# Attention value product: three query groups per head pair joined to two, with the output transposes moved later

## The chip, the cores and the metric

One Trainium2 chip; the kernel runs on one core. The metric is device microseconds (us) of one execution. The engines of a core run side by side and meet only at semaphores: PE (TensorE: matmul, and transpose as a matmul against an identity), PEld (its weight loads), DVE (VectorE), ACT (ScalarE), POOL (GpSimd) and SP (SyncE, which here issues the DMA transfers).

## The reference

Three layers in a row: an attention with pooled queries, a soft mixture of experts, and a gated feed-forward layer. Only the first is touched.

```
B, H, S, D = q.shape                      # 4, 8, 1152, 64
q_pool = q.reshape(B, H, S // 2, 2, D).mean(axis=3)        # 576 queries a head
scores = scale * np.matmul(q_pool, k.transpose(0, 1, 3, 2))  # 576 x 1152
scores = scores - np.max(scores, axis=-1, keepdims=True)
attn = np.exp(scores)
attn = attn / (np.sum(attn, axis=-1, keepdims=True) + 1e-09)
return np.matmul(attn, v).astype(np.float32)               # 576 x 64
```

What follows (2304 tokens of 512 features through the experts and the feed-forward layer) reads the whole attention output.

## The kernel before

The 32 heads are worked off as 16 pairs of heads. A pair has 2 x 576 queries. Eight score tiles hold 128 queries of one head each; the ninth holds the last 64 queries of both heads. So `NTILE` is 9, and one pass over a pair (`pair`) has nine periods, t = 0 to 8, of three chunks j = 0 to 2. In this document (t, j) is a chunk, and a prime, as in (0', 2), means the next pair's pass.

PE's order is written out by hand in `pair` (the loop that calls `job`, `score_chunk` and `weighted`). In each chunk it does

- `job`: three 128 x 128 transposes of a softmax tile that is two periods old, into one of two PSUM banks of `tbank` that all jobs take in turn; a job waits until the job two before it has been copied out;
- `score_chunk`: the scores of the tile of period t against 384 keys, two matmuls (four in period 8, whose tile has queries of both heads). Chunk 0 waits for the exponential of tile t - 2, chunk 2 for that of tile t - 1;
- in chunk 1 only, an extra job of the table `EXTRA`: K0, K1, Q0 and KQ transpose keys and queries of the next pair; O0 (four transposes) and O1 (one) transpose the finished output of the pair before;
- in chunk 1 only, after that, a burst of value matmuls (`weighted`) of the table `PV`.

DVE copies the transposed probabilities of chunk 1 to the tile `pt` (or `pt_tail`), divides what O0 and O1 transposed by the row sums into `x_nat` (`normalise`, lines 852 and 856), and takes the row maxima of the scores: one pass over chunks 0 and 1 (`maxima`, line 806), one over chunk 2 (`maxima_end`, line 813). ACT copies the probabilities of chunks 0 and 2 (line 746), takes the exponential of the tile of the period before (`softmax_exp`, line 718), and copies finished value sums from the PSUM bank `obank` to `o_t` (`copy_group`, line 733). In period 3 DVE has four small operations more (`inverses`).

The value product of a pair, transposed, is (64 values x 576 queries) for each head; the two heads lie in partitions 0 to 63 and 64 to 127 of `obank`. It is done in three groups of queries: group 0 (256 queries), group 1 (256) and group 2 (the last 64). Each sums over nine key tiles, so it takes 18 matmuls in the program, and as the data is plain 32-bit float each of them is two matmul instructions in the trace: 36 a group. A group is spread over several periods. `PV` counts periods through: 6, 7, 8 are periods of the pair itself, 9 to 14 are periods 0 to 5 of the next pair's pass. There is one `obank`: the first burst of a group waits until ACT has copied the group before out, and until the last transposed tile that it needs has been copied to `pt`.

One cycle of value work therefore runs from period 6 of a pair to period 5 of the next pair's pass. After the last pair there is one more pass (`ends=(NPAIR,)`) without scores, here called the drain. It does the last two transposed tiles, the rest of the last pair's value work, O0 and O1. Then a barrier for all engines ends the phase, and the experts begin.

The keys and queries of the next pair reach the score matmuls by DMA copies (`stack`) that SP issues after KQ has been worked up by ACT and POOL; the scores of (0', 0) wait for the first head's copies, those of (1', 0) for the second's.

Of the kernel before, what the change touches and what calls it, by code (L numbers as in the profile page):

```python
# [6 lines left out]
P = 128  # L7
FP32 = mybir.dt.float32
# [78 lines left out]

EXTRA = {(1, 1): "K0", (2, 1): "K1", (3, 1): "Q0", (4, 1): "KQ", (5, 1): "O0", (7, 1): "O1"}  # L90
PREPS = ("K0", "K1", "Q0", "KQ")
PREP_BY_ACT = ("K0", "K1", "Q0", "KQ")
JOBS = []
# [33 lines left out]
def in_range(pair, k):  # L127
# [2 lines left out]

PV = {6: (0, (0, 1, 2)), 7: (0, (3, 4)), 8: (0, (5, 6)), 9: (0, (7, 8)),
      10: (1, (0, 1, 2)), 11: (1, (3, 4, 5)), 12: (1, (6, 7, 8)),
      13: (2, (0, 1, 2, 3, 4)), 14: (2, (5, 6, 7, 8))}

s_scores = Stream(3 * NTILE, in_range)
s_tiles = Stream(NTILE, in_range)
s_jobs = Stream(len(JOBS), job_exists)
s_by_act = Stream(len(JOBS), lambda p, k: job_exists(p, k) and job_by_act(k))  # L140
s_by_dve = Stream(len(JOBS), lambda p, k: job_exists(p, k) and not job_by_act(k))
s_groups = Stream(3, in_range)


def previous_user(at, k, back=2):
# [22 lines left out]
def attention(nc, mem, q, k, v):  # L168
# [24 lines left out]
    v_in = sb("v_in", [P, 2, 2, NK * D], FP32)  # L193
    probs = sb("probs", [P, 2, S], FP32)
    pt_at = mem.at
    pt = sb("pt", [P, 2, 2, NK, 2 * P], FP32)
    pt_tail = sb("pt_tail", [P, NK, P], FP32)
    o_t = sb("o_t", [P, 2, SQ], FP32)
    one = sb("one", [P, 1], FP32)
    row_max = sb("row_max", [P, 2, 2], FP32)  # L200
# [9 lines left out]
    mem.at = pt_at + 4 * 2 * NK * 2 * P  # L210
    q_parts = sb("q_parts", [P, 2, NI, 3, D], F32R)
    q_total = sb("q_total", [P, 2, NI, D], FP32)
    assert mem.at <= pt_at + 4 * 4 * NK * 2 * P
    mem.at = after_pt
    scores = ps("scores", [P, 5, 512])
    tbank = ps("tbank", [P, 2, 512])
# [166 lines left out]
    @block.sync  # L383
    def _(sp):
        def load_keys(at, ahead):
            par = (at.pair + ahead) % 2
            two = bass.ds(at.index(ahead) * 2, 2)
            if at.pair + ahead == 1:
                sp.wait_ge(q_parts_v, 2)
                sp.wait_ge(q_parts_p, 3)  # L390
            else:
                for h in range(2):
                    sp.dma_start(k_in[:, par, :, h, :], k_v[:, bass.ds(at.index(ahead) * 2 + h, 1)].rearrange(
                        "p n j d -> p (n j) d")).then_inc(k_loaded[par], 16)
                sp.wait_ge(q_pooled, pooled(at, ahead - 1))
            sp.dma_start(q_in[:, :, 0:NF, :].rearrange("p h i m -> p h (i m)"),
                         q_full[:, two, :]).then_inc(q_loaded[par], 16)
            sp.dma_start(q_in[0:TAIL, :, NF, :], q_tail[:, two, :]).then_inc(q_loaded[par], 16)

        def load_values(at, ahead):  # L400
            par = (at.pair + ahead) % 2
            two = bass.ds(at.index(ahead) * 2, 2)
            sp.dma_start(v_in[:, par], v_v[:, two, :]).then_inc(v_loaded[par], 16)

        for h in range(2):
            sp.dma_start(k_stage[:, h].rearrange("p j d -> p (j d)"), k_v[:, h].rearrange("p j d -> p (j d)")
                         ).then_inc(k_staged[h], 16)
            sp.dma_start(q_in[:, h, 0:NF, :].rearrange("p i m -> p (i m)"),
                         q_full[:, h, :]).then_inc(q_loaded[0] if h else q_first_in, 16)
        sp.dma_start(q_in[0:TAIL, :, NF, :], q_tail[:, 0:2, :]).then_inc(q_loaded[0], 16)  # L410
        for h in range(2):
            sp.dma_start(k_in[:, 1, :, h, :], k_v[:, 2 + h]).then_inc(k_loaded[1], 16)
        load_keys(At(0), 1)
        load_values(At(0), 0)
        load_values(At(0), 1)

        def body(at):
            last = extra_at("KQ")
            if at.pair + 2 < NPAIR:

                if at.pair >= 1:
                    sp.wait_ge(job_ready, s_jobs.count(at, 1, last))
                load_keys(at, 2)
            if at.pair + 1 < NPAIR:


                sp.wait_ge(lo_ready, split_count(at, 1, "KQ"))
                stack(sp, at, 1)
                if at.pair >= 1:

                    sp.wait_ge(group_ready, s_groups.count(at, 1, 2))
                    load_values(at, 1)
            if at.step is None and at.pair == 1:
                for n in range(EARLY):
                    mem.load_weight(sp, n)

        each_pair(sp, body)

        for par in range(2):
            for h in range(2):  # L440
                sp.wait_ge(stacked[par][h], 16 * HEAD_DMAS[h] * (NPAIR // 2 - (par == 0)))
        mem.load_weight(sp, 2)

        sp.wait_ge(scores_ready, 3 * NTILE * (NPAIR - 1))
        mem.load_weight(sp, 3)
        mem.load_weight(sp, 4)
        sp.wait_ge(scores_ready, 3 * NTILE * NPAIR)
        mem.load_weight(sp, 5)
# [47 lines left out]
    def _(pe):  # L496
# [5 lines left out]
        def job(at, k):  # L502
            kind, period, j = JOBS[k]
            if not job_exists(at.pair, k):
                return
            user = previous_user(at, k)

            if user is not None:
                back, e = user
                if job_by_act(e):  # L510
                    pe.wait_ge(out_by_act, s_by_act.count(at, back, e))
                else:
                    pe.wait_ge(out_by_dve, s_by_dve.count(at, back, e))
            elif bank_of(at, k):
                pe.wait_ge(first_by_act, 5)
            else:
                pe.wait_ge(first_by_dve, 1)
            if kind == "main" and j == 0:
                back, t = tile_of(at.pair, period)
                pe.wait_ge(exp_done, s_tiles.count(at, back, t))  # L520
            if kind == "K0":
                pe.wait_ge(k_loaded[(at.pair + 1) % 2], loads(at, 1) * 32)
            if kind == "Q0":
                pe.wait_ge(q_pooled, pooled(at, 1))
            if kind == "O0":
                pe.wait_ge(group_out, s_groups.count(at, 1, 1))
            if kind == "O1":
                pe.wait_ge(group_out, s_groups.count(at, 1, 2))
            transposes(at, k, bank_of(at, k))

        def score_chunk(at, t, c):
# [35 lines left out]
        def weighted(at, back, group, tiles):  # L567
# [3 lines left out]
            par = (at.pair - back) % 2  # L571
            if tiles[0] == 0:

                last_tile = (3, 7, 8)[group]
                period = last_tile + 2
                b2, per = (back, period) if period < NTILE else (back - 1, period - NTILE)
                for j in (1, 2):
# [3 lines left out]
                    else:  # L581
                        pe.wait_ge(out_by_dve, s_by_dve.count(at, b2, e))

                g = 3 * (at.pair - back) + group
                if g >= 1:
                    b3, gg = (back, group - 1) if group else (back + 1, 2)
                    pe.wait_ge(group_out, s_groups.count(at, b3, gg))
                else:
                    pe.wait_ge(first_by_dve, 7)
                if group == 0:  # L590
                    pe.wait_ge(v_loaded[par], (uses(at, -back)) * 16)
            for kt in tiles:
                for h in range(2):
                    rows = slice(D * h, D * h + D)
                    if group < 2:
                        rhs, cols = pt[:, group, h, kt, :], slice(0, 2 * P)
                    else:
                        rhs, cols = pt_tail[:, kt, TAIL * h:TAIL * h + TAIL], slice(0, TAIL)
                    last = nc.tensor.matmul(obank[rows, cols], v_in[:, par, h, D * kt:D * kt + D],  # L599
                                            rhs, start=(kt == 0), stop=(kt == NK - 1))  # L600
            if tiles[-1] == NK - 1:
                last.then_inc(group_ready, 1)

# [72 lines left out]
    def pt_out(at, k):  # L676

        _, period, j = JOBS[k]
        back, t = tile_of(at.pair, period)
        parity = (NTILE * (at.pair - back) + t) % 2  # L680
        first = key_tile(parity, 3 * j)
        if t == 2 * NF:
            return pt_tail[:, first:first + 3, :]
        i, h = divmod(t, 2)
        return pt[:, i // 2, h, first:first + 3, P * (i % 2):P * (i % 2) + P]

    def pt_free(engine, at, k):

        _, period, j = JOBS[k]
        back, t = tile_of(at.pair, period)  # L690
        group = 2 if t == 2 * NF else t // 4
        if at.pair - back >= 1:
            engine.wait_ge(group_ready, s_groups.count(at, back + 1, group))

# [1 line left out]
    def _(act):  # L696
# [26 lines left out]
        def copy_group(at, back, group):  # L723
# [5 lines left out]

            if group == 0 and at.pair - back >= 2:  # L730
                act.wait_ge(job_ready, s_jobs.count(at, back + 1, extra_at("O1")))
            first, n = ((0, 2 * P), (2 * P, 2 * P), (NF * P, TAIL))[group]
            nc.scalar.copy(o_t[:, par, first:first + n], obank[:, 0:n]).then_inc(group_out, 1)

        def pair(at):
            for t in range(NTILE):

                for period, back, group in ((1, 1, 0), (4, 1, 1), (6, 1, 2)):
                    if t == period:
                        copy_group(at, back, group)  # L740
                for j in range(3):
                    e = JOBS.index(("main", t, j))
                    if job_exists(at.pair, e) and job_by_act(e):
                        act.wait_ge(job_ready, job_count(at, e))
                        pt_free(act, at, e)
                        nc.scalar.copy(pt_out(at, e), tbank[:, bank_of(at, e), 0:3 * P].rearrange(  # L746
                            "p (r q) -> p r q", r=3)).then_inc(out_by_act, 1)
                    if j == 0:

                        softmax_exp(at, *((0, t - 1) if t else (1, NTILE - 1)))  # L750
# [11 lines left out]
    def _(dve):  # L762
# [98 lines left out]
        def pair(at):  # L861
            for t in range(NTILE):
                for j in range(3):
                    e = JOBS.index(("main", t, j))
                    if job_exists(at.pair, e) and not job_by_act(e):
                        dve.wait_ge(job_ready, job_count(at, e))
                        pt_free(dve, at, e)
                        nc.vector.tensor_copy(pt_out(at, e), tbank[:, bank_of(at, e), 0:3 * P].rearrange(  # L868
                            "p (r q) -> p r q", r=3)).then_inc(out_by_dve, 1)
                    if (t, j) in EXTRA:  # L870
                        kind = EXTRA[t, j]
                        e = JOBS.index((kind, t, j))
# [1060 lines left out]
```

## Time and profile before

| | us |
|---|---|
| median of 3 runs | 820.52 |
| lowest, highest | 820.22, 822.13 |
| the profiled execution | 822.02 |
| its span, first to last instruction | 820.0 |
| PE busy in the span | 795.1 |
| DVE busy | 497.2 |
| ACT busy | 462.4 |
| POOL busy | 182.9 |

In the timeline below, a row merges neighbouring instructions of one kind: start, duration from the first start to the last end, engine, line, operation, tiles, shape, count. In square brackets stand the idle time of the engine before the row and what ended it. The ends of matmuls overlap what follows, so the cost of a piece of PE work is read from its start to the start of the next row, not from its duration.

### The profile page before, as it was taken

Reading aid. Unit: us, or ns where it says so; the run is one execution under the profiler, and the core shown is the slowest. Engines: PE = TensorE matmul, PEld = TensorE weight load, DVE = VectorE, ACT = ScalarE, POOL = GpSimd, SP = SyncE. Lnnn points to the kernel's source line nnn. Section 1 sums busy time; section 2 is a strip of 40 time slices with the busy share of each in tenths; the row PEclk is TensorE's granted clock in tenths of the full one; section 3 lists DMA queues with packets and bytes.
Section 4 is the critical chain, followed back from the end, with each engine's and each line's share of the span. In section 5 each row is a group of like instructions: output and inputs, shape, how many; then the busy total and the mean of one; then the engine's idle time right before and its main releaser. Section 6 shows DMA issues by size and latency. Waiting matters only on the chain. (4 is left out here: it accounts for less than half of the span.)

```text
span 820.0 us, 17518 instructions
## 1 busy us (share of the span) xinstructions
PE 795.1 (97%) x5858; PEld 606.6 (74%) x5858; DVE 497.2 (61%) x968; ACT 462.4 (56%) x889; POOL 182.9 (22%) x246
## 2 busy tenths in 40 slices
PE   8999999999999999999999999998799999999997
PEld 7777777777777777777777777765334788888886
DVE  6666657657566666665765766743323566666665
ACT  5676666767666667666676766642123453343333
POOL 4541331513315225133151330000002330000000
PEclk9999999999999999999999999999799899999999
DMA  5738856374382553734637417639799001010110
GB/s 150 182 80 260 225 122 158 78 169 105 96 197 63 143 124 85 194 86 116 158 78 166 107 39 198 255 112 394 301 393 392 5 1 52 0 52 1 51 52 26
DMA packets 83033, 112.05 MB, mean 137 GB/s; under 512 B 45360, under 2 KB 47408, under 8 KB 82480
## 3 DMA queue, kind: packets, MB, share of 16 engines
q1 hardware_dynamic: 82832, 111.24, 47.6%
q8 instruction: 26, 0.43, 0.2%
q10 hardware_dynamic: 160, 0.26, 0.1%
q14 instruction: 15, 0.12, 0.0%
HBM read 71.37 MB, written 4.72 MB: 93 GB/s over the span
## 5 line engine op out<-in xcount | busy, mean ns | idle before, releaser
L562 PE MATMUL scores<-k_stack,q_stack 128*128 128x384 f32 x960 | 275.1, 376 | 2.3 <-DVE q_stack L777 1.2
L499 PE MATMUL tbank<-ident,probs 128*128 128x128 f32 x1296 | 219.6, 278 | 2.8 <-DVE pt L868 2.4
L746 ACT COPY pt<-tbank 128x384 f32<-128x384 f32 x256 | 122.7, 479 | 143.9 <-PE tbank L499 142.7
L499 PEld LDWEIGHTS tbank<-ident,probs 128*128 128x128 f32 x1296 | 156.4, 140 | 58.7 <-issue 40.4
L718 ACT ACTIVATE probs<-scores,neg_max 128x1152 f32<-128x1152 f32 x144 | 175.9, 1221 | 6.5 <-PE tbank L499 2.1
L813 DVE TENSOR_REDUCE row_max<-scores 128x1 f32<-128x384 f32 x144 | 80.0, 556 | 130.1 <-PE scores L562 128.2
L562 PEld LDWEIGHTS scores<-k_stack,q_stack 128*128 128x128 f32 x960 | 147.9, 191 | 3.7 <-ACT k_stack L372 1.6
L599 PE MATMUL obank<-pt,v_in 128*64 128x256 f32 x1152 | 148.8, 389 | 0.0
L806 DVE TENSOR_REDUCE row_max<-scores 128x1 f32<-128x768 f32 x144 | 136.7, 949 | 4.4 <-PE scores L562 1.7
L599 PEld LDWEIGHTS obank<-pt,v_in 128*64 128x64 f32 x1152 | 72.8, 136 | 49.3 <-issue 23.5
L337 POOL TENSOR_TENSOR k_hi<-k_lo,one 128x512 fp32r<-128x512 f32 (+1 forms) x45 | 37.2, 826 | 291.4 <-ACT k_lo L670 270.8
L1698 ACT CAST h_hi<-hid 128x512 fp32r<-128x512 f32 (+1 forms) x60 | 34.7, 578 | 101.2 <-DVE hid L1835 101.2
L868 DVE COPY pt<-tbank 128x384 f32<-128x384 f32 x128 | 71.3, 557 | 32.0 <-PE tbank L499 28.7
L1601 PE MATMUL banks<-wo_hi,h_hi 128*128 128x512 f32 x216 | 85.8, 397 | 0.6 <-DVE h_lo L1841 0.4
L1601 PE MATMUL banks<-wo_lo,h_hi 128*128 128x512 f32 x216 | 84.7, 392 | 0.0
L1601 PE MATMUL banks<-wo_hi,h_lo 128*128 128x512 f32 x216 | 84.5, 391 | 0.0
L1841 DVE TENSOR_TENSOR h_lo<-hid,h_hi 128x512 fp32r<-128x512 f32 (+1 forms) x60 | 38.3, 639 | 37.9 <-ACT h_hi L1698 37.9
L1786 DVE TENSOR_TENSOR scaled<-banks,inv_rms 128x512 f32<-128x512 f32 (+1 forms) x60 | 38.2, 636 | 26.7 <-PE banks L1513 26.0
L1601 PEld LDWEIGHTS banks<-wo_hi,h_hi 128*128 128x128 f32 x216 | 40.9, 190 | 11.3 <-DVE h_lo L1841 3.2
L1601 PEld LDWEIGHTS banks<-wo_hi,h_lo 128*128 128x128 f32 x216 | 40.8, 189 | 8.7
L1601 PEld LDWEIGHTS banks<-wo_lo,h_hi 128*128 128x128 f32 x216 | 40.9, 189 | 8.0
L342 POOL TENSOR_TENSOR k_lo<-k_lo,k_hi 128x512 fp32r<-128x512 f32 (+1 forms) x45 | 45.1, 1003 | 3.5
(220 smaller groups left out, 773.6 us busy)
## 6 DMA issues: line engine op xcount, KB each, us to landing
weights<-in_moe_w SPq DMA_DIRECT2D x7, 2048.0 KB, 9.4
v_in<-in_v SPq DMA_DIRECT2D x16, 576.0 KB, 3.9
k_in<-in_k SPq DMA_DIRECT2D x30, 288.0 KB, 4.8
k_stack<-k_hi SPq DMA_DIRECT2D x30, 288.0 KB, 3.7
k_stack<-k_lo SPq DMA_DIRECT2D x30, 288.0 KB, 3.6
q_in<-in_q SPq DMA_DIRECT2D x15, 512.0 KB, 4.7
slots_of_four<-in_moe_w SPq DMA_DIRECT2D x12, 512.0 KB, 11.2
q_stack<-q_hi SPq DMA_DIRECT2D x30, 144.0 KB, 3.3
```

Of the source, the lines that this page charges most:

```text
L342: last = ops.tensor_tensor(low[:, cols], low[:, cols].bitcast(FP32), high[:, cols].bitcast(FP32), ALU.subtract)
L499: last = nc.tensor.transpose(tbank[:, bank, cols], src, ident[0:rows, 0:rows])
L562: last = nc.tensor.matmul(scores[:, bank, 0:CH], q_stack[at.par][:, h, order, cols], k_stack[at.par][:, h, keys], start=(x == 0), stop=(x ...
L599: last = nc.tensor.matmul(obank[rows, cols], v_in[:, par, h, D * kt:D * kt + D], rhs, start=(kt == 0), stop=(kt == NK - 1))
L718: nc.scalar.activation(probs[:, odd, :].rearrange("p (c k) -> p c k", c=3), scores[:, first:first + 3, 0:CH], ACT.Exp, bias=neg_max[:, odd ...
L746: nc.scalar.copy(pt_out(at, e), tbank[:, bank_of(at, e), 0:3 * P].rearrange("p (r q) -> p r q", r=3)).then_inc(out_by_act, 1)
L806: nc.vector.tensor_reduce(row_max[:, odd, 0:1], scores[:, first:first + 2, 0:CH], axis=AX.XY, op=ALU.max).then_inc(partial_max, 1)
L813: nc.vector.tensor_reduce(row_max[:, odd, 1:2], scores[:, 2, 0:CH], axis=AX.X, op=ALU.max).then_inc(partial_max, 1)
L868: nc.vector.tensor_copy(pt_out(at, e), tbank[:, bank_of(at, e), 0:3 * P].rearrange("p (r q) -> p r q", r=3)).then_inc(out_by_dve, 1)
L1601: last = nc.tensor.matmul(y_ps[:, t, :], a[:, f % 3, cols], w[:, f, :], start=(f == 0 and x == 0), stop=(f == NFT - 1 and x == 2))
L1786: nc.vector.tensor_tensor(scaled[:, f % 2, 0:width], gv_ps[:, f % 2, 0, 0:width], inv_rms[:, columns(n)], ALU.mult).then_inc(scaled_done, 1)
L1841: nc.vector.tensor_tensor(h_lo[:, f % 3, 0:width], hid2[:, f % 2, 0:width], h_hi[:, f % 3, 0:width].bitcast(FP32), ALU.subtract).then_inc( ...
```

## The change

Groups 1 and 2 become one: group 1 now has 320 queries (the former 256 and the last 64), and its matmuls are 320 columns wide. The tile `pt_tail` goes; the probabilities of the last 64 queries are copied to the last 64 columns of group 1's tile, so that the copy out of `tbank` writes two 64-column pieces a key tile instead of 128 columns in a row. ACT copies two groups a pair out of `obank` (256 and 320 columns) instead of three, in periods 2 and 6 instead of 1, 4 and 6. O0 moves from period 5 to 7, O1 from 7 to 8. The bursts are laid out anew:

| period | before: group, matmul instructions | after |
|---|---|---|
| 6 | 0, 12 | 0, 12 |
| 7 | 0, 8 | 0, 8 |
| 8 | 0, 8 | none |
| 0' | 0, 8 | 0, 8 |
| 1' | 1, 12 | 0, 8 |
| 2' | 1, 12 | 1, 12 of 320 columns |
| 3' | 1, 12 | 1, 8 of 320 columns |
| 4' | 2, 20 of 64 columns | 1, 8 of 320 columns |
| 5' | 2, 16 of 64 columns | 1, 8 of 320 columns |

```diff
-EXTRA = {(1, 1): "K0", (2, 1): "K1", (3, 1): "Q0", (4, 1): "KQ", (5, 1): "O0", (7, 1): "O1"}
+EXTRA = {(1, 1): "K0", (2, 1): "K1", (3, 1): "Q0", (4, 1): "KQ", (7, 1): "O0", (8, 1): "O1"}
...
-PV = {6: (0, (0, 1, 2)), 7: (0, (3, 4)), 8: (0, (5, 6)), 9: (0, (7, 8)),
-      10: (1, (0, 1, 2)), 11: (1, (3, 4, 5)), 12: (1, (6, 7, 8)),
-      13: (2, (0, 1, 2, 3, 4)), 14: (2, (5, 6, 7, 8))}
+PV = {6: (0, (0, 1, 2)), 7: (0, (3, 4)), 9: (0, (5, 6)), 10: (0, (7, 8)),
+      11: (1, (0, 1, 2)), 12: (1, (3, 4)), 13: (1, (5, 6)), 14: (1, (7, 8))}
+GROUP_FIRST, GROUP_WIDTH = (0, 2 * P), (2 * P, 2 * P + TAIL)
...
-    pt = sb("pt", [P, 2, 2, NK, 2 * P], FP32)
-    pt_tail = sb("pt_tail", [P, NK, P], FP32)
+    pt = [sb(f"pt{g}", [P, 2, NK, GROUP_WIDTH[g]], FP32) for g in range(2)]
...
-                last_tile = (3, 7, 8)[group]
+                last_tile = (3, NTILE - 1)[group]
...
-                    if group < 2:
-                        rhs, cols = pt[:, group, h, kt, :], slice(0, 2 * P)
-                    else:
-                        rhs, cols = pt_tail[:, kt, TAIL * h:TAIL * h + TAIL], slice(0, TAIL)
-                    last = nc.tensor.matmul(obank[rows, cols], v_in[:, par, h, D * kt:D * kt + D],
-                                            rhs, start=(kt == 0), stop=(kt == NK - 1))
+                    last = nc.tensor.matmul(obank[rows, 0:GROUP_WIDTH[group]], v_in[:, par, h, D * kt:D * kt + D],
+                                            pt[group][:, h, kt, :], start=(kt == 0), stop=(kt == NK - 1))
...
         if t == 2 * NF:
-            return pt_tail[:, first:first + 3, :]
+            return pt[1][:, :, first:first + 3, 2 * P:2 * P + TAIL].rearrange("p h r q -> p r h q")
...
-                for period, back, group in ((1, 1, 0), (4, 1, 1), (6, 1, 2)):
+                for period, back, group in ((2, 1, 0), (6, 1, 1)):
```

The waits on group 2 become waits on group 1; the rest of the diff counts groups as two instead of three.

## Rows read from the trace of the kernel before

**Rows 1.** The page's busy time of each engine, share of the span, instructions.

```profile
PE 795.1 (97%) x5858; PEld 606.6 (74%) x5858; DVE 497.2 (61%) x968; ACT 462.4 (56%) x889; POOL 182.9 (22%) x246
```

**Rows 2.** All of PE's waits, 60 to 525 us: total, times, longest.

```profile
PE tbank L499 <- DVE pt L868: 2.4, 12, 0.2
```

**Rows 3.** Timeline of PE, period 0' to chunk (1', 0) of the first cycle.

```profile
39.60 0.49 PE L499 MATMUL tbank<-ident,probs 128*128 128x128 f32 x3
40.28 0.49 PE L499 MATMUL tbank<-ident,probs 128*128 128x128 f32 x3
...
42.81 0.49 PE L499 MATMUL tbank<-ident,probs 128*128 128x128 f32 x3
43.75 0.62 PE L562 MATMUL scores<-k_stack,q_stack 128*128 128x384 f32 x2 [0.45 <-DMA q_stack<-q_lo]
```

**Rows 4.** Timeline of PE, periods 4 to 8 of a later pass.

```profile
223.71 0.80 PE L599 MATMUL obank<-pt_tail,v_in 128*64 128x64 f32 x20
224.71 0.55 PE L499 MATMUL tbank<-ident,probs 128*128 128x128 f32 x3 [0.20 <-DVE pt L868]
...
226.82 0.60 PE L499 MATMUL tbank<-ident,o_t 128*128 128x128 f32 x4
...
230.15 1.51 PE L599 MATMUL obank<-pt,v_in 128*64 128x256 f32 x12
231.60 0.55 PE L499 MATMUL tbank<-ident,probs 128*128 128x128 f32 x3
...
233.70 0.27 PE L499 MATMUL tbank<-ident,o_t 128*128 128x128 f32 x1
233.90 1.08 PE L599 MATMUL obank<-pt,v_in 128*64 128x256 f32 x8
234.92 0.55 PE L499 MATMUL tbank<-ident,probs 128*128 128x128 f32 x3
...
235.66 0.49 PE L499 MATMUL tbank<-ident,probs 128*128 128x128 f32 x3
...
236.69 0.49 PE L499 MATMUL tbank<-ident,probs 128*128 128x128 f32 x3
```

**Rows 5.** Timeline of DVE and ACT in the same stretch.

```profile
227.59 0.69 DVE L852 TENSOR_TENSOR x_nat<-tbank,row_inv 128x512 f32 x1 [0.37 <-PE tbank L499]
...
234.14 0.29 DVE L856 TENSOR_TENSOR x_nat<-tbank,tail_inv 64x128 f32 x1
234.46 0.96 DVE L806 TENSOR_REDUCE row_max<-scores 128x1 f32<-128x768 f32 x1
...
235.86 0.56 DVE L813 TENSOR_REDUCE row_max<-scores 128x1 f32<-128x384 f32 x1 [0.44 <-PE scores L562]
236.19 0.48 ACT L746 COPY pt<-tbank 128x384 f32<-128x384 f32 x1 [0.20 <-PE tbank L499]
...
236.70 1.22 ACT L718 ACTIVATE probs<-scores,neg_max 128x1152 f32<-128x1152 f32 x1
...
237.21 0.56 DVE L868 COPY pt<-tbank 128x384 f32<-128x384 f32 x1 [0.55 <-PE tbank L499]
...
237.82 0.19 ACT L718 ACTIVATION_READ_ACCUMULATOR probs<-scores,neg_max 128x1 f32 x1
```

**Rows 6.** Timeline of all engines in the drain.

```profile
540.93 1.52 PE L599 MATMUL obank<-pt,v_in 128*64 128x256 f32 x12
...
545.71 0.37 ACT L733 COPY o_t<-obank 128x256 f32<-128x256 f32 x1 [2.27 <-PE obank L599]
...
546.23 0.80 PE L599 MATMUL obank<-pt_tail,v_in 128*64 128x64 f32 x20 [0.56 <-ACT o_t L733]
546.96 0.66 PE L499 MATMUL tbank<-ident,o_t 128*128 128x128 f32 x4
547.72 0.69 DVE L852 TENSOR_TENSOR x_nat<-tbank,row_inv 128x512 f32<-128x512 f32 x1 [5.44 <-PE tbank L499]
548.97 0.29 DVE L856 TENSOR_TENSOR x_nat<-tbank,tail_inv 64x128 f32<-64x128 f32 x1 [0.56 <-PE tbank L499]
```

More of the change, by code:

```diff
@@ L141 @@
 s_by_dve = Stream(len(JOBS), lambda p, k: job_exists(p, k) and not job_by_act(k))
-s_groups = Stream(3, in_range)
+s_groups = Stream(2, in_range)
 def previous_user(at, k, back=2):
@@ L212, in attention @@
     q_total = sb("q_total", [P, 2, NI, D], FP32)
-    assert mem.at <= pt_at + 4 * 4 * NK * 2 * P
+    assert mem.at <= pt_at + 4 * 2 * NK * (2 * P + 2 * P + TAIL)
     mem.at = after_pt
@@ L429, in body @@
                 if at.pair >= 1:
-                    sp.wait_ge(group_ready, s_groups.count(at, 1, 2))
+                    sp.wait_ge(group_ready, s_groups.count(at, 1, 1))
                     load_values(at, 1)
@@ L527, in job @@
             if kind == "O1":
-                pe.wait_ge(group_out, s_groups.count(at, 1, 2))
+                pe.wait_ge(group_out, s_groups.count(at, 1, 1))
             transposes(at, k, bank_of(at, k))
@@ L582, in weighted @@
                         pe.wait_ge(out_by_dve, s_by_dve.count(at, b2, e))
-                g = 3 * (at.pair - back) + group
+                g = 2 * (at.pair - back) + group
                 if g >= 1:
-                    b3, gg = (back, group - 1) if group else (back + 1, 2)
+                    b3, gg = (back, 0) if group else (back + 1, 1)
                     pe.wait_ge(group_out, s_groups.count(at, b3, gg))
@@ L682, in pt_out, with pt_from @@
         if t == 2 * NF:
-            return pt_tail[:, first:first + 3, :]
+            return pt[1][:, :, first:first + 3, 2 * P:2 * P + TAIL].rearrange("p h r q -> p r h q")
         i, h = divmod(t, 2)
-        return pt[:, i // 2, h, first:first + 3, P * (i % 2):P * (i % 2) + P]
+        return pt[i // 2][:, h, first:first + 3, P * (i % 2):P * (i % 2) + P]
+    def pt_from(at, k):
+        cells = tbank[:, bank_of(at, k), 0:3 * P]
+        if tile_of(at.pair, JOBS[k][1])[1] == 2 * NF:
+            return cells.rearrange("p (r h q) -> p r h q", r=3, h=2)
+        return cells.rearrange("p (r q) -> p r q", r=3)
     def pt_free(engine, at, k):
@@ L690, in pt_free @@
         back, t = tile_of(at.pair, period)
-        group = 2 if t == 2 * NF else t // 4
+        group = min(t // 4, 1)
         if at.pair - back >= 1:
@@ L731, in copy_group @@
                 act.wait_ge(job_ready, s_jobs.count(at, back + 1, extra_at("O1")))
-            first, n = ((0, 2 * P), (2 * P, 2 * P), (NF * P, TAIL))[group]
+            first, n = GROUP_FIRST[group], GROUP_WIDTH[group]
             nc.scalar.copy(o_t[:, par, first:first + n], obank[:, 0:n]).then_inc(group_out, 1)
@@ L745, in pair @@
                         pt_free(act, at, e)
-                        nc.scalar.copy(pt_out(at, e), tbank[:, bank_of(at, e), 0:3 * P].rearrange(
-                            "p (r q) -> p r q", r=3)).then_inc(out_by_act, 1)
+                        nc.scalar.copy(pt_out(at, e), pt_from(at, e)).then_inc(out_by_act, 1)
                     if j == 0:
@@ L867, in pair @@
                         pt_free(dve, at, e)
-                        nc.vector.tensor_copy(pt_out(at, e), tbank[:, bank_of(at, e), 0:3 * P].rearrange(
-                            "p (r q) -> p r q", r=3)).then_inc(out_by_dve, 1)
+                        nc.vector.tensor_copy(pt_out(at, e), pt_from(at, e)).then_inc(out_by_dve, 1)
                     if (t, j) in EXTRA:
```

## Prediction

> **What bounds the kernel now.** I read the page's busy times first. PE is busy 97% of the span, DVE 61%, ACT 56% [rows 1]. A busy PE need not be an unbroken one, so I then asked for PE's waits over the 465 us in which the passes are all alike: 12 waits of 0.2 us, 2.4 us together, all for one DVE copy [rows 2]. The reader is to see what is not there: no wait for ACT, POOL or DMA. DVE and ACT wait for PE instead (the idle times in [rows 5] end with PE). So until the drain the time is the sum of PE's own work in its written order, and an edit is worth what it takes from that order, plus that wait, unless it creates a wait. Last I read PE's timeline, where work is measured from start to start, and the drain, where PE does wait.
>
> **The change part by part.**
>
> *Cost of a burst.* A chunk of three transposes and two score matmuls takes 0.68 us without a burst (39.60 to 40.28 [rows 3]). Chunks (0, 1) and (0, 2) with a burst of 8 between them take 40.28 to 42.81 = 2.53 us [rows 3]; less 2 x 0.68, that burst costs 1.17 us. One of 12 lasts 230.15 to 231.60 = 1.45, one of 8 233.90 to 234.92 = 1.02 [rows 4]: 0.1075 us for each further 256-column matmul. So a burst costs 1.17 - 8 x 0.1075 = 0.31 us beside its matmuls, 0.16 of it inside the burst (1.02 - 8 x 0.1075). Eight bursts instead of nine: -0.31 us a cycle.
>
> *Cost of the columns.* The tail's burst of 20 lasts 546.23 to 546.96 = 0.73 us [rows 6], so a 64-column matmul costs (0.73 - 0.16) / 20 = 0.0285. The trace has no 320-column matmul. On the line through the 64- and 256-column values it costs 0.1075 + 64 x (0.1075 - 0.0285) / 192 = 0.134. I take that: it is the same operation on the same operands. The lower end is 0.1075 (the 64 columns for nothing). For the upper end I take the worst column rate on this engine: period 8's chunk, with two more 384-column score matmuls, takes 235.66 to 236.69 = 1.03 [rows 4] against 0.68, so 0.175 each, which gives 0.146 for 320. With 36 instructions of each kind: 36 x (0.1075 + 0.0285 - 0.134) = 0.07 us less a cycle, between 1.0 less and 0.36 more.
>
> *Cycles.* 15 full cycles (the 16th ends in the drain): 15 x (0.31 + 0.07) = 5.7 us less.
>
> *The wait that goes.* In period 4 the tail's burst takes 223.71 to 224.71 = 1.00 us instead of 0.73, because chunk (4, 2) waits for DVE's copy of (4, 1), late behind DVE's extra operations of period 3 [rows 4]. After, the burst there is 8 matmuls of 320 columns, 8 x 0.134 + 0.16 = 1.23 us, longer than what DVE needs, so the wait is covered. 12 waits [rows 2] x 0.27 = 3.2 us less. What is late next is nothing on PE: the next exponential has the longer bursts of periods 4 and 5 as cover.
>
> *O0 and O1 moved.* Four transposes and one take the same PE time wherever a burst or a chunk follows; their row durations, 0.60 and 0.27 [rows 4], differ by 0.11 us a transpose. But period 8 loses its burst, the cover for DVE's work, and DVE's longer division (0.69 us, 227.59) takes the place of the short one (0.29, 234.14) just before [rows 5]. Followed with the trace's times: the burst of period 7 starts 0.33 later, (7, 2) at 235.25, (8, 0) at 235.99, (8, 1) at 237.02. With no burst (8, 2) follows after 1.03 + 0.11, at 238.16, and can score after its three transposes, at 238.40; its scores need the exponential of tile 7. DVE divides O0 from 234.47 to 235.16 (0.77 after the transposes, as at 226.82 and 227.59), takes the maxima to 236.13 and reaches the second pass at 236.19, when the scores of (7, 2) are ready (235.86 + 0.33). The exponential starts 0.84 later (as 236.70 after 235.86), at 237.03, and is through 1.31 later (237.82 + 0.19 - 236.70), at 238.34. ACT's copy of (8, 0) moves by the same 0.33 and is out of its way. That is 0.06 us ahead of need. The copy of (8, 1) that (8, 2) needs ends at 238.10, also 0.06 ahead. O1's division then pushes the maxima of tile 8; the same steps give its exponential at 241.92, and (0', 2) needs it at 241.97. Three margins of 0.05 us are less than the hand-over between engines is known to. I charge 0.07 us a cycle: 15 x 0.07 = 1.0 us more. The lower end is 0; the upper is 0.40, by which O0's division is longer than O1's, were nothing of it hidden: 6.0 us.
>
> *The first cycle.* Here chunk (1', 0) waits 0.45 us for the stacked queries of pair 1 [rows 3]; they come from work done before the first value burst, which the change leaves where it is. PE arrives there 1.17 us earlier (period 8 has no burst) and waits that much longer: +1.2 us. Later passes have no such wait [rows 2].
>
> *Copies.* ACT's copy of 64 columns goes and one of 256 grows to 320; ACT has idle time there. The tail's copies write 64-column pieces. No row shows that shape; at 0.48 (ACT, 236.19) and 0.56 us (DVE, 237.21) [rows 5] for the same 384 elements I cost the change at nothing, from 0.1 less up to a doubling, which DVE's one copy a pass could show at most as 0.56 us in period 1', where an 8-burst of 1.02 lies over it. No DMA is issued earlier or later in SP's order; the value load waits, as before, for the last burst of period 5.
>
> *The drain.* Up to (8, 2) PE is 0.33 - 1.02 = 0.69 us earlier, but tile 8's exponential, which the drain's transposes wait for, only some 0.36 (O1's division lies before it). Then a burst of 8 of group 0 stands where the first of group 1 stood: 540.93 - 0.36 = 540.57 to 541.59. Group 1 now waits until ACT has copied the last transposes (0.48, 0.58 after they start, as for (8, 0)) and group 0 (0.37): to 543.02, and a hand-over of 0.15 (546.08 to 546.23 [rows 6]) makes 543.17. 36 x 0.134 = 4.82 us to 547.99; ACT's copy, 0.26 later and 0.43 long (an estimate from 0.37 for 256 columns), to 548.68; O0 at 548.83, its division 0.76 later (546.96 to 547.72) and 0.69 long, O1's 0.29: 550.6. Before, the end is 548.97 + 0.29 = 549.26 [rows 6]. +1.4 us. The barrier behind it moves by the same, and the phases after it rigidly.
>
> *Sum.* -5.7 - 3.2 + 1.0 + 1.2 + 1.4 = -5.3 us. The profiled execution took 822.02 us (span 820.0), so it becomes 816.7; the median of the runs, 1.5 lower, goes from 820.5 to 815.2.
>
> **A rule against the row.** The tail burst of 20 in 0.73 us [rows 6] holds 20 weight loads as well, so hardly any of a load shows. The Trainium skill ("TensorE: Matmul & The Clock Gate", section "Part 3: Packing small matmuls — row/col tiling") says that a weight load overlaps matmuls in flight only when its row group differs; here all loads use all 128 rows. By that rule and the page's load time, 53 ns for 64 columns (an estimate), dropping 36 loads a cycle would give 1.9 us a cycle, near 30 us in all. The trace disagrees: 0.0285 us a matmul is less than such a load.
>
> **The rivals.**
> (A) *Period 8 becomes bound by DVE and ACT.* The chain maxima, exponential, scores of (8, 2) ends after PE. For it: the margins above. Against: in [rows 5] DVE still waits 0.44 us for PE at 235.86, so O0's extra 0.40 just fits. If 0.25 to 0.40 us shows in each cycle, the time is 817.9 to 820.2.
> (B) *Wide matmuls cost more than their columns.* 320 columns could run like 384, 0.1075 x 1.5 = 0.161. That is 0.027 x 36 = 0.97 us a cycle, over 16 cycles 15.6: 830.8, slower. It turns slower from 0.148 on ((0.1475 - 0.134) x 576 = 7.8 us leads to 823.0), which the score matmuls' rate of 0.146 nearly reaches. Against it: those carry 128-column weights of another type, and 64 and 256 columns of the same operation lie on one line with almost no offset.
> (C) *The wait in period 4 stays*, since DVE, not PE, sets that time. For it: DVE's lateness is unchanged. Against: the new burst is 0.23 us longer than the old one with its wait. Time 815.2 + 3.2 = 818.4.
> (D) *The weight loads that go are worth time.* Even if the last 64 queries came free, the gain would be 36 x 0.0285 = 1.03 us a cycle instead of 0.07, 15.4 us more: 799.8. The short tail matmuls speak against it.
>
> **How the numbers follow.** A measurement here can tell about 0.3%, 2.5 us, from no change: below 818.0 is faster, above 823.0 slower. My forecast 815.2, with its own range 812.5 to 817.5 (a first cycle, drain and stalls that cost 2.7 us less or 2.3 more): 0.72. More gain than that, D with it: 0.05. A: 0.11, of which 0.04 below 818.0. C: 0.06, half of it on either side. B: 0.06, slower. So faster 0.72 + 0.05 + 0.04 + 0.03 = 0.84, same 0.07 + 0.03 = 0.10, slower 0.06. The range reaches up to the lower part of A and to C: 812.3 to 818.5.
>
> **What would show it.** In the changed profile: 320-column matmuls 0.134 us apart (B if 0.146 or more); a cycle 0.65 us shorter; no wait of (4, 2) for DVE (C if it is there); at (8, 2) and (0', 2) waits for ACT of at most 0.1 us each (A if 0.25); a wait for DMA near 1.6 us at the first (1', 0); 1.3 us more from the drain's last group to the barrier. The prediction is wrong if waits of PE that are not listed here come up in every pass.

## The result and the profile after

The changed kernel takes 814.61 us (median of 4 runs, 813.68 to 815.96) against 820.89 for the kernel before on the same chip: a ratio of 0.9917, 95% interval 0.9896 to 0.9937. Forecast were 815.2 us and a gain of 5.3; it is faster by 6.3. The profiled execution took 815.96 us, 6.06 less than the one before.

The page of the changed kernel, busy time of each engine (after [rows 1]):

```profile
PE 788.2 (97%) x5282; PEld 586.0 (72%) x5282; DVE 499.2 (61%) x968; ACT 460.9 (57%) x873; POOL 183.2 (23%) x246
```

576 matmul instructions fewer, 36 for each of 16 cycles, and PE as busy as before. The view of PE's waits from 60 to 525 us ([rows 2]) has no entry left. PE's timeline: two period-7 bursts one pass apart (199.64 and 232.34), the burst before chunk (4, 2), and chunks (8, 1) and (8, 2):

```profile
199.64 1.08 PE L594 MATMUL obank<-pt,v_in 128*64 128x256 f32 x8
...
221.42 1.30 PE L594 MATMUL obank<-pt,v_in 128*64 128x320 f32 x8
222.65 0.55 PE L498 MATMUL tbank<-ident,probs 128*128 128x128 f32 x3
...
232.34 1.08 PE L594 MATMUL obank<-pt,v_in 128*64 128x256 f32 x8
...
235.12 0.49 PE L498 MATMUL tbank<-ident,probs 128*128 128x128 f32 x3
235.37 0.95 PE L561 MATMUL scores<-k_stack,q_stack 128*128 128x384 f32 x4
236.15 0.27 PE L498 MATMUL tbank<-ident,o_t 128*128 128x128 f32 x1
236.26 0.55 PE L498 MATMUL tbank<-ident,probs 128*128 128x128 f32 x3
236.56 0.94 PE L561 MATMUL scores<-k_stack,q_stack 128*128 128x384 f32 x4
```

DVE, ACT and PEld (PE's weight loads) in the same stretches:

```profile
222.03 0.56 DVE L869 COPY pt<-tbank 128x384 f32<-128x384 f32 x1 [0.19 <-DVE tail_inv L838]
...
222.64 0.31 PEld L498 LDWEIGHTS tbank<-ident,probs 128*128 128x128 f32 x3 [0.49 <-DVE pt L869]
...
234.29 0.56 DVE L814 TENSOR_REDUCE row_max<-scores 128x1 f32<-128x384 f32 x1 [0.16 <-PE scores L561]
...
235.65 0.56 DVE L869 COPY pt<-tbank 128x384 f32<-128x384 f32 x1 [0.55 <-PE tbank L498]
...
236.25 0.19 ACT L720 ACTIVATION_READ_ACCUMULATOR probs<-scores,neg_max 128x1 f32 x1
236.26 0.31 PEld L498 LDWEIGHTS tbank<-ident,probs 128*128 128x128 f32 x3
```

A pass is 32.70 us; before it was 33.29. The 8-burst of 320 columns takes 1.23 us, as forecast, and PE loses nothing behind it (before: 1.00 with the wait, [rows 4]). But the cover is only just long enough: DVE's copy of (4, 1) ends at 222.59, 1.17 us after the burst began, and the weight load of (4, 2) that needs it starts 0.05 us later, just when the burst is over.

At (8, 2) the step from transposes to scores is 0.30 us, where (8, 1) has 0.25. These 0.05 us are not the exponential of tile 7. It is through at 236.44, 0.12 us before the scores; in the kernels below whose scores do wait for it, they start 0.05 us after its end. The cause is DVE's copy of (8, 1): with O1's job in between, (8, 2) takes the bank of (8, 1), and the weight load of its first transpose starts at 236.26, 0.05 us after that copy ends (236.21), as at (4, 2).

PE's timeline shortly after the first bursts, the answer to the last two of [rows 3]:

```profile
42.52 0.49 PE L498 MATMUL tbank<-ident,probs 128*128 128x128 f32 x3
44.58 0.62 PE L561 MATMUL scores<-k_stack,q_stack 128*128 128x384 f32 x2 [1.57 <-DMA q_stack<-q_lo]
...
49.90 1.84 PE L594 MATMUL obank<-pt,v_in 128*64 128x320 f32 x12
51.66 0.55 PE L498 MATMUL tbank<-ident,probs 128*128 128x128 f32 x3
```

The wait for the DMA grew from 0.45 to 1.57 us. Over the whole trace a burst of 12 takes 1.77 us on average, a burst of 8 1.23: 0.134 us for each further 320-column matmul. The drain, all engines (after [rows 6]):

```profile
533.49 1.08 PE L594 MATMUL obank<-pt,v_in 128*64 128x256 f32 x8
...
535.47 0.38 ACT L735 COPY o_t<-obank 128x256 f32<-128x256 f32 x1
...
535.99 5.07 PE L594 MATMUL obank<-pt,v_in 128*64 128x320 f32 x36 [0.94 <-ACT o_t L735]
541.09 0.42 ACT L735 COPY o_t<-obank 128x320 f32<-128x320 f32 x1 [5.25 <-PE obank L594]
...
541.66 0.74 PE L498 MATMUL tbank<-ident,o_t 128*128 128x128 f32 x5 [0.61 <-ACT o_t L735]
542.40 0.69 DVE L853 TENSOR_TENSOR x_nat<-tbank,row_inv 128x512 f32<-128x512 f32 x1 [7.55 <-PE tbank L498]
543.12 0.29 DVE L857 TENSOR_TENSOR x_nat<-tbank,tail_inv 64x128 f32<-64x128 f32 x1
...
543.74 2.48 PE L1035 MATMUL banks<-ident,x_nat 128*128 128x128 f32 x21 [1.34 <-PEq L1885]
```

The spans, 820.02 and 813.95 us, cut at instructions of PE that both kernels have:

| stretch | before, us | after, us | difference |
|---|---|---|---|
| start to the first value burst | 29.94 | 30.70 | +0.76 |
| to the scores of pair 2 | 43.75 | 43.41 | -0.34 |
| 13 passes, to the scores of pair 15 | 432.62 | 425.08 | -7.54 |
| to the first matmul of the next phase | 43.28 | 44.55 | +1.27 |
| the next phases | 270.43 | 270.21 | -0.22 |

The first row is no part of the change, whose first edit lies behind it. The same load lands later in this execution, and PE, which waits for it, falls below its upper level of 2.4 GHz. DVE's timeline and the busy times with the granted clock (the column after POOL) of the changed kernel:

```profile
7.87 0.23 DVE L349 TENSOR_TENSOR q_total<-q_in 128x64 f32<-128x64 f32 x1 [2.41 <-DMA q_in<-in_q]
```

```profile
8.00:12.00 4.00, 2.90 (x11) 2.83 (x12) 3.05 (x8) 0.12 (x1) 3.21 (x7) 0.65 0.09 18
```

Before, DVE waited 1.56 us there and the clock was 1.00. In the ten traces of this document the first value burst starts at 29.50 to 30.70 us and the next phases take 267.3 to 271.4, though no edit touches either. So for each kernel below I also give what the change can touch, from the first value burst to the first matmul of the next phase, called the core: 519.65 us before, 513.04 after, 6.61 less.

### The profile page after: what moved, and what is told of

The parts are those of the page before. It is cut to its first block and busy times, and to the rows that moved or that the text cites. A ratio compares the mean times of both kernels' runs of the same rounds, so it can differ in the third digit from the quotient of the medians.

```text
span 814.0 us, 16310 instructions
## 1 busy us (share of the span) xinstructions
PE 788.2 (97%) x5282; PEld 586.0 (72%) x5282; DVE 499.2 (61%) x968; ACT 460.9 (57%) x873; POOL 183.2 (23%) x246
## 5 line engine op out<-in xcount | busy, mean ns | idle before, releaser
L748 ACT COPY pt<-tbank 128x384 f32<-128x384 f32 x288 | 138.2, 480 | 153.7 <-PE tbank L498 153.7
L594 PE MATMUL obank<-pt,v_in 128*64 128x320 f32 (+1 forms) x1152 | 167.3, 417 | 0.9 <-ACT o_t L735 0.9
L869 DVE COPY pt<-tbank 128x384 f32<-128x384 f32 x144 | 80.2, 557 | 39.0 <-PE tbank L498 36.4
```

The source lines that it names most:

```text
L594: last = nc.tensor.matmul(obank[rows, 0:GROUP_WIDTH[group]], v_in[:, par, h, D * kt:D * kt + D], pt[group][:, h, kt, :], start=(kt == 0), ...
L748: nc.scalar.copy(pt_out(at, e), pt_from(at, e)).then_inc(out_by_act, 1)
L869: nc.vector.tensor_copy(pt_out(at, e), pt_from(at, e)).then_inc(out_by_dve, 1)
```

## Experiments

The theory: PE's written order is the time. A burst less gains 0.31 us a cycle less what the uncovered chain of DVE and ACT takes back in period 8, the covered wait 0.27, the columns 0.07. Rivals: the joined group carries the gain; DVE has room anyway; moving the outputs costs or gains by itself. A pass is the mean of nine, from pair 3 to pair 12.

| kernel | pass, us | core, us | median, us | ratio to before (95%) |
|---|---|---|---|---|
| before | 33.29 | 519.65 | 821.77, 821.65 | |
| early row sums | 33.02 | 516.14 | 818.96 | 0.9961 (0.9945 to 0.9977) |
| eight bursts | 32.96 | 516.91 | 819.43 | 0.9974 (0.9959 to 0.9989) |
| both of these | 32.86 | 515.75 | 816.89 | 0.9948 (0.9928 to 0.9967) |
| changed, nine bursts | 33.08 | 518.62 | 818.9 | 0.9977 (0.9963 to 0.9991) |
| changed, again | 32.70 | 512.91 | 813.86 | 0.9902 (0.988 to 0.9924) |
| changed, divided twice | 32.87 | 516.14 | 818.14 | 0.9954 (0.9937 to 0.997) |
| changed, outputs one earlier | 32.78 | 514.13 | 815.56 | 0.9928 (0.9905 to 0.995) |
| changed, ends mended | 32.71 | 511.19 | 812.9 | 0.9896 (0.9873 to 0.9919) |

The first four beside 30 runs of before, the last four on another chip beside 15.

**The wait alone.** The kernel before, with

```diff
-                if t == 3:
+                if t == 2:
                     inverses(at)
```

> The kernel before, with one edit: DVE's four small operations on the row sums run in period 2 instead of 3. Theory (PE's wait of 0.27 us in period 4 comes from these operations alone, and PE is the bound, so the wait is worth what it lasts): no wait of chunk (4, 2) for DVE is left, a pass is 33.0 instead of 33.3 us, and the time is 3.2 to 3.6 us less than before. Rival (DVE's lateness only moves: the copy it delays in period 3, or the next exponential, holds PE up instead): no gain, and another wait of some 0.2 us a pass.

PE's timeline at period 4:

```profile
223.13 0.80 PE L599 MATMUL obank<-pt_tail,v_in 128*64 128x64 f32 x20
223.87 0.55 PE L499 MATMUL tbank<-ident,probs 128*128 128x128 f32 x3
```

The burst takes 0.74 us instead of 1.00; the core is 3.51 us shorter, as expected, and the median 2.8, somewhat less. Half of what the change gained is to be had by moving one call, without joining anything.

**The burst alone.** The kernel before, with

```diff
-PV = {6: (0, (0, 1, 2)), 7: (0, (3, 4)), 8: (0, (5, 6)), 9: (0, (7, 8)),
-      10: (1, (0, 1, 2)), 11: (1, (3, 4, 5)), 12: (1, (6, 7, 8)),
+PV = {6: (0, (0, 1, 2)), 7: (0, (3, 4)), 9: (0, (5, 6)), 10: (0, (7, 8)),
+      11: (1, (0, 1, 2, 3, 4)), 12: (1, (5, 6, 7, 8)),
...
-                for period, back, group in ((1, 1, 0), (4, 1, 1), (6, 1, 2)):
+                for period, back, group in ((2, 1, 0), (4, 1, 1), (6, 1, 2)):
```

> The kernel before, still with three groups and 64-column tail matmuls, but with eight bursts instead of nine: none in period 8; group 0 in 6, 7, 0', 1' (12, 8, 8, 8 instructions), group 1 in 2' and 3' (20 and 16), tail as before; ACT copies group 0 in period 2. Theory (a burst costs 0.31 us beside its matmuls): 15 x 0.31 = 4.7 us less, the first cycle's DMA wait 1.2 us more, the drain some 1.0 more: 2.5 us less than before; the wait of (4, 2) for DVE stays, and a pass is 33.0 us. Rival (a burst costs only its matmuls, and the gain of the change came from the wider matmuls): no gain in a pass, 2.2 us more in all.

The core is 2.74 us shorter, as expected, but by two errors that cancel. The wait did not stay: the burst of 20 takes 0.82 us, so 0.18 of the wait is gone. And the burst gained less than 0.31. The next run tells how much.

**Both.**

> The two edits of the experiments before together: three groups with 64-column tail matmuls, eight bursts, the operations on the row sums in period 2. Theory (the change gained by a burst less and a wait less; the joined group itself is worth 0.07 us a cycle): 5.5 to 6.1 us less than before, within 1.5 us of the changed kernel (814.6); a pass is 32.7 to 32.8 us. Rival (the joined group carries the gain): the changed kernel stays 3 us or more ahead of this.

Missed: 32.86 us a pass, the core 3.90 us shorter and the median 4.9, not 5.5 to 6.1. Against the early row sums alone the burst brings 0.16 us a pass. PE's timeline at (8, 2), with the end of ACT's exponential of tile 7, shows what takes the rest:

```profile
202.90 0.49 PE L499 MATMUL tbank<-ident,probs 128*128 128x128 f32 x3
203.15 0.94 PE L562 MATMUL scores<-k_stack,q_stack 128*128 128x384 f32 x4
...
203.93 0.49 PE L499 MATMUL tbank<-ident,probs 128*128 128x128 f32 x3
204.03 0.19 ACT L718 ACTIVATION_READ_ACCUMULATOR probs<-scores,neg_max 128x1 f32 x1
...
204.28 0.96 PE L562 MATMUL scores<-k_stack,q_stack 128*128 128x384 f32 x4
```

The step from transposes to scores is 0.25 us in (8, 1) and 0.35 in (8, 2): 0.10 us of waiting for the exponential of tile 7, which ends 0.05 us before the scores. Here O1 is transposed in period 7, so PE reaches (8, 2) 0.11 us sooner, and waits. The changed kernel's core is 2.71 us shorter than this one's, between what the two theories said: the joined group with the later outputs is worth more than I thought, though less than the rival needs.

**A ninth burst.** The changed kernel, with

```diff
-PV = {6: (0, (0, 1, 2)), 7: (0, (3, 4)), 9: (0, (5, 6)), 10: (0, (7, 8)),
+PV = {6: (0, (0, 1, 2)), 7: (0, (3, 4)), 8: (0, (5, 6)), 9: (0, (7,)), 10: (0, (8,)),
```

> The changed kernel with a ninth burst: group 0 in periods 6, 7, 8, 0', 1' (12, 8, 8, 4, 4 instructions). Theory (0.31 us a burst): a cycle of 33.0 instead of 32.7 us, 15 x 0.31 = 4.7 us more, the first cycle's DMA wait 0.7 less: 4.0 us more than the changed kernel, 2.3 less than before. Rival (bursts cost only their matmuls): the same time as the changed kernel.

0.38 us more a pass, the core 5.6 more. The rival is out: the matmuls are the same. But not all of it is the burst. Averaged over the passes, the chunk with the burst of period 8 grows by some 0.25 us more than its matmuls; the rest, some 0.14, is the chain once more, behind the short burst of period 0'. PE's timeline:

```profile
208.32 0.65 PE L594 MATMUL obank<-pt,v_in 128*64 128x256 f32 x4
208.90 0.55 PE L498 MATMUL tbank<-ident,probs 128*128 128x128 f32 x3
209.36 0.62 PE L561 MATMUL scores<-k_stack,q_stack 128*128 128x384 f32 x2
```

From transposes to scores 0.46 us, where [rows 4] and the trace after have 0.30 behind a burst (222.65 to 222.95): 0.16 us of waiting, in every second pass; in those between it is 0.08. A burst costs itself, and gives back what the chain would have made PE wait without it.

**The changed kernel again**, beside the next three.

> The changed kernel as it is, beside the next three on the same chip. Both theories: 6 to 7 us less than before, a pass of 32.70 us.

7.8 us less than before by the medians, a little over the range; pass and core as in the first execution.

**More work for DVE in period 7.** The changed kernel, with

```diff
+                nc.vector.tensor_tensor(
+                    spare[:], tbank[:, bank, :].rearrange("p (i h d) -> p i h d", i=NF, h=2),
+                    inv.unsqueeze(3).broadcast_to([P, NF, 2, D]), ALU.mult).then_inc(spare_done, 1)
                 nc.vector.tensor_tensor(
                     x_pair[:, 0:NF], tbank[:, bank, :].rearrange("p (i h d) -> p i h d", i=NF, h=2),
```

> The changed kernel with DVE's division of O0 in period 7 done twice, the first time into a spare tile: 0.69 us more of DVE work before the maxima of tile 7. Theory (without a burst in period 8 the chain maxima, exponential, scores of (8, 2) runs level with PE; DVE's idle 0.16 us before its second pass of tile 7 is all that is left): some 0.5 us of it shows at (8, 2), a pass of 33.2 us, 15 x 0.5 = 7.5 us more than the changed kernel. Rival (DVE, busy 61%, has room for it): the time stays.

0.17 us a pass, not 0.5, and 3.2 us in the core. The rival is out, but my size was wrong. DVE's and PE's timelines:

```profile
199.83 0.69 DVE L855 TENSOR_TENSOR spare<-tbank,row_inv 128x512 f32<-128x512 f32 x1 [0.23 <-PE tbank L500]
200.44 0.68 DVE L858 TENSOR_TENSOR x_nat<-tbank,row_inv 128x512 f32 x1
201.04 0.95 DVE L809 TENSOR_REDUCE row_max<-scores 128x1 f32<-128x768 f32 x1
201.90 0.55 DVE L816 TENSOR_REDUCE row_max<-scores 128x1 f32<-128x384 f32 x1
```

```profile
203.65 0.55 PE L500 MATMUL tbank<-ident,probs 128*128 128x128 f32 x3
204.10 0.97 PE L563 MATMUL scores<-k_stack,q_stack 128*128 128x384 f32 x4
```

DVE's rows overlap: each starts 0.08 to 0.09 us before the one ahead of it ends, so an operation in a queue costs less than its row's duration, here 0.61 for 0.69 and 0.86 for 0.95. DVE's idle 0.16 us before its second pass (234.29 in the changed kernel) is used up, and the first division starts earlier: 0.63 us after O0's transposes instead of 0.77. So the second pass comes only 0.22 us later after the start of (7, 2). Of that, 0.07 was to spare, as the exponential was through 0.12 us before the scores where 0.05 is enough. The rest, 0.15, is what (8, 2) now waits for the exponential: 0.45 us from transposes to scores instead of 0.30.

**The outputs one period earlier.**

```diff
-(7, 1): "O0", (8, 1): "O1"}
+(6, 1): "O0", (7, 1): "O1"}
```

> The changed kernel with O0 in period 6 and O1 in period 7, one period earlier each. Theory (PE's order decides; but O1's transpose in period 8 fills 0.11 us in which PE would wait for the exponential of tile 7): PE waits up to 0.1 us more at (8, 2), a pass of 32.70 to 32.80 us, the drain 0.3 us shorter: from 0.3 less to 1.3 us more than the changed kernel. Rival (moving the outputs by two periods cost something through DVE in periods 7 and 8): 1 us or more faster than the changed kernel, a shorter pass.

0.08 us more a pass, as expected; the core is 1.2 us longer than the changed kernel's, the median 1.7, and the drain did not get shorter. PE's timeline shows 0.35 us from the transposes of (8, 2) to its scores, so PE waits 0.10 for the exponential, as in the experiment with both edits:

```profile
203.62 0.49 PE L498 MATMUL tbank<-ident,probs 128*128 128x128 f32 x3
203.97 0.97 PE L561 MATMUL scores<-k_stack,q_stack 128*128 128x384 f32 x4
```

O0's and O1's transposes cost PE the same in either place (the chunk of period 6 grows by 0.43 us, those of 7 and 8 shrink by 0.32 and 0.11); what is left is (8, 2), 1.16 us instead of 1.09. The run also isolates the join: this kernel and the one with both edits have the same number of bursts and the same wait at (8, 2), and differ by 0.08 us a pass, against 0.07 forecast for the columns. (O0 and DVE's row-sum operations stand in other periods in the two, but no wait of PE in the passes comes from that.)

**The ends mended.** The changed kernel, with

```diff
+PV_FIRST = {6: (0, (0, 1, 2)), 7: (0, (3, 4)), 8: (0, (5, 6)), 9: (0, (7, 8)),
+            11: (1, (0, 1, 2)), 12: (1, (3, 4)), 13: (1, (5, 6)), 14: (1, (7, 8))}
...
+            final = at.pair == NPAIR and group == 1
+            sums = scores[:, 0, :] if final else obank
...
+                    if at.pair == NPAIR and (t, j) == (1, 2):
+                        weighted(at, 1, 1, (0, 1, 2))
+                        weighted(at, 1, 1, (3, 4, 5, 6, 7, 8))
```

> The changed kernel with its two ends mended: the first pair keeps a burst in period 8 (bursts 6, 7, 8, 0', then none in 1'), and in the drain the last group 1 sums in a bank of the scores that is free by then and starts with key tiles 0 to 2 without waiting for ACT's copies of the last chunk and of group 0. Theory: the wait for DMA at the first (1', 0) shrinks from 1.6 to 0.4 us (1.2 us less), PE's wait of 0.9 us in the drain goes (0.9 to 1.0 less): 2.0 us less than the changed kernel, the same 32.70 us pass. Rival (the ends are hidden behind the next phase's DMA, or PE waits elsewhere for the same transfers): the time of the changed kernel.

PE's timeline at the two ends:

```profile
43.50 0.62 PE L563 MATMUL scores<-k_stack,q_stack 128*128 128x384 f32 x2 [0.52 <-DMA q_stack<-q_lo]
...
533.05 5.07 PE L603 MATMUL scores<-pt,v_in 128*64 128x320 f32 x36
```

The DMA wait is 0.52 us and the last group starts without one. The core is 1.72 to 1.85 us shorter than the changed kernel's, as the theory has it; the medians, 812.9 and 813.86, agree in sign, but their intervals overlap. By the trace it is the fastest of these kernels.

## Why the prediction was right

**The bound, and the steps in a pass.** PE's order was the time: each edit's price came out of PE's timeline. Of the pass I forecast -0.31 - 0.07 - 0.27 + 0.07 = -0.58 us (the signs that I listed have 0.65, without the chain's 0.07); measured -0.59. Each term by itself: the wait 0.27 (early row sums), the columns 0.08 (0.134 us a matmul, as forecast), and the burst 0.38 with the ninth put back, of which some 0.14 is the chain's. That leaves 0.25 for the burst, where I had 0.31 less 0.07 for the chain; without the 0.05 us at (8, 2) in the changed kernel it would be 0.30. So these 0.05 us are about what I had charged, but not where I looked first: of the margins of 0.06 that I had worked out, the exponential's held, and the copy's did not, because I had counted from the transposes and not from the weight load ahead of them, which is what waits. That charge came out by luck, since I could not tell it from nothing.

**A cover that held by luck.** I had the new burst of period 4, 1.23 us, as longer than what DVE needs, which was 1.00 before. But DVE needed 1.22 in the changed kernel (221.42 to 222.64), as one of its small operations took 0.56 us instead of 0.33 (the last section shows why). The wait went, with next to nothing to spare.

**What I had not seen.** The outputs' move pays. I took the later O0 and O1 as a risk for DVE. But O1's transpose, in period 8, is work that PE does while it would wait for the exponential; with it back in period 7 the pass is 0.08 longer. Together with the 0.08 of the columns that makes the 0.16 us a pass by which taking the wait and the burst from the kernel before falls short of the change, most of the 2.7 us of the core, where I had expected 1.5 at most.

**Sizes.** The core gained 6.6 us, not 5.3. The drain cost 0.95 us (from the last pair's period-6 burst to the next phase, 21.77 before and 22.72 after), not 1.4: group 0's burst in the drain came 0.64 us earlier (12.47 after that burst instead of 13.11), not 0.36, because DVE's second pass in the last pair did not wait as long behind O1's division as I counted; and ACT's last two copies overlap by 0.10. The wait was worth 3.5 us (early row sums), not 3.2: I had counted the 12 waits in the view and not two shorter ones, 0.12 us each, in pairs 1 and 14. The DMA wait grew by 1.12, against 1.2.

**The rivals.** A (the chain takes over) is not there in the changed kernel: the exponential is 0.07 us ahead of need. It is close, though: PE waits 0.10 us for it with the outputs one period earlier, 0.15 with a second division. B fell with 0.134. C fell, narrowly: no wait of PE is left in period 4. D fell, and with it the reading of the Trainium skill's rule on weight loads ("TensorE: Matmul & The Clock Gate", section "Part 3: Packing small matmuls — row/col tiling") that I weighed: the loads that went were worth at most what the columns' term holds, 0.08 us a cycle.

**Still open.** The 0.76 us at the start and up to some 4 us between executions in the last phases (267.3 to 271.4 us over these traces), which no edit touched, were not looked into beyond the one load above.

## What to carry to other kernels

Where one engine is without waits, price an edit by the steps from start to start on that engine: a burst there cost some 0.25 to 0.31 us beside its matmuls, and fusing two groups was worth far less (0.08) than having a burst less. Such a step can hold a wait shorter than those that the view of waits lists, so compare it with the same step elsewhere, and compare the end of each candidate with the start that it should hold up: 0.05 us apart was a wait here, 0.12 was not. Before a piece of work is taken from such an engine, look at the chain beside it: the piece was cover, and a small independent operation moved into the gap (0.11 us of transpose) can pay for itself. And look for the wait that is one moved call away; it was half of this gain.

## What the runs showed of the hardware

A DVE operation of nine values waited for POOL. The row-sum addition takes 0.16 us in the eight-burst kernel, 0.33 in the kernel before and 0.56 in the changed one; these three timelines show why, before, changed, and eight bursts:

```profile
221.98 1.28 POOL L342 TENSOR_TENSOR q_lo<-q_lo,q_hi 128x512 fp32r<-128x512 f32 x1
...
222.96 0.33 DVE L831 TENSOR_SCALAR row_sum_eps<-row_sum 128x9 f32<-128x9 f32 x1
```

```profile
219.91 1.29 POOL L341 TENSOR_TENSOR q_lo<-q_lo,q_hi 128x512 fp32r<-128x512 f32 x1
...
220.67 0.56 DVE L832 TENSOR_SCALAR row_sum_eps<-row_sum 128x9 f32<-128x9 f32 x1
```

```profile
220.48 1.28 POOL L342 TENSOR_TENSOR q_lo<-q_lo,q_hi 128x512 fp32r<-128x512 f32 x1
...
221.89 0.16 DVE L831 TENSOR_SCALAR row_sum_eps<-row_sum 128x9 f32<-128x9 f32 x1
```

In the first two it ends 0.03 us after POOL's operation ends (223.29 and 223.26; 221.23 and 221.20); in the third it starts 0.13 us after POOL is done. It is the same in each of the 14 passes of each of the three, and in the last two passes, without an operation of POOL beside it, the addition takes 0.16 or 0.17 us in all three. The Trainium skill ("SBUF — State Buffer", section "Who interferes with whom") says that a DVE operation that uses both of its port pairs, as a TENSOR_SCALAR can, shares one of them with POOL, and that whoever comes first holds it for the whole instruction. The traces agree, as POOL came first. So these two engines meet here without a semaphore between them, and 0.17 of the 0.27 us of PE's wait in the kernel before was POOL's doing, which explains why the wait shrank by 0.18 in the eight-burst kernel, where POOL's operation lies earlier against DVE's.
